# Two index lists in one tile of 96 bytes, and the buffers behind it on multiples of 128 bytes

## The reference

```python
for t in range(S):
    state = alpha[:, :, t, :, None] * state + np.einsum('bhd,bhe->bhde', k[:, :, t], v[:, :, t])
    y[:, :, t] = np.einsum('bhd,bhde->bhe', q[:, :, t], state)
...
for e in range(E):
    mask = expert_idx == e
    h = np.maximum(x[mask] @ w1[e], 0.0)          # 384 -> 1024
    out[mask] = gate_w[mask, None] * (h @ w2[e])  # 1024 -> 384
...
h = x @ w_in                                      # 384 -> 2048
g = np.maximum(0.01 * h, h)
return (g @ w_out).astype(np.float32)             # 2048 -> 384
```

## Time and profile before

| | us |
|---|---|
| median of 3 runs (lowest, highest) | 817.68 (817.54, 819.99) |
| span of the profiled execution, first to last instruction | 817.2 |
| TensorE matmul busy | 801.6 (98%) |
| VectorE, ScalarE, GpSimd busy | 452.1, 346.0, 209.0 |
| TensorE granted clock, share of full speed | 0.998 |

### The profile page before, as it was taken

How to read it: one execution, slowest core, us unless ns; L and a number is a source line. 1 busy time by engine, 2 the same in 40 slices (tenths; PEclk the granted TensorE clock), 3 DMA queues, 4 the chain that set the end, 5 groups by cost and what they waited for, 6 DMA issues and landing times.

```text
span 817.2 us, 17577 instructions
## 1 busy us (share of the span) xinstructions
PE 801.6 (98%) x5259; PEld 719.7 (88%) x5260; DVE 452.1 (55%) x705; ACT 346.0 (42%) x643; POOL 209.0 (26%) x278
## 2 busy tenths in 40 slices
PE   7899999999999999999999999999999999999998
PEld 7788887889989989999889988889998888998987
DVE  7899987686577476566565334433433533433332
ACT  3455554565446256444443333332333333334223
POOL 6567632223343343341241021003003001001000
PEclk9999999999999999999999999999999999999999
DMA  9988762777887887897741110201201001000001
GB/s 222 256 250 248 219 225 85 265 231 278 301 290 250 283 271 225 291 312 228 201 45 21 20 39 1 40 1 39 39 0 39 0 0 39 1 1 20 20 1 39
DMA packets 64130, 108.98 MB, mean 133 GB/s; under 512 B 24199, under 2 KB 45747, under 8 KB 64080
## 3 DMA queue, kind: packets, MB, share of 16 engines
q1 hardware_dynamic: 54896, 93.47, 37.7%
q0 software_dynamic: 5888, 14.85, 5.8%
q10 hardware_dynamic: 3296, 0.06, 0.2%
HBM read 78.89 MB, written 30.85 MB: 134 GB/s over the span
## 4 chain that ended last, share of the span: by engine, by line
PE 90%; DVE 3%; DMA 3%; issue 2%; POOL 1%; ACT 0%; DVEq 0%; ACTq 0%; SPq 0%; POOLq 0%
PE bank L1772 25%; PE bank L1721 24%; PE bank L1694 15%; PE bank L1674 14%; DMA qkas<-qka 2%; PE bank L1516 2%; PE bank L1556 2%; PE bank L1533 2%; PE bank L1564 1%; PE bank L1650 1%; PE bank L1522 1%; PE bank L1576 1%; POOL kt L675 1%; DVE decay L1073 0%; DMA xg<-x_rows,slot_src 0%
## 5 line engine op out<-in xcount | busy, mean ns | idle before, releaser
L1721 PE MATMUL bank<-yT,wts 128*128 128x512 f32 x864 | 217.5, 395 | 0.3 <-DVE yT L1306 0.3
L1772 PE MATMUL bank<-wts,gs 128*128 128x384 f32 x1152 | 215.5, 335 | 0.4 <-ACT os L1023 0.2
L1772 PEld LDWEIGHTS bank<-wts,gs 128*128 128x128 f32 x1152 | 202.0, 188 | 10.9 <-issue 2.0
L1721 PEld LDWEIGHTS bank<-yT,wts 128*128 128x128 f32 x864 | 160.6, 188 | 31.4 <-DVE yT L1306 1.0
L1302 DVE TENSOR_TENSOR g<-bank,small 128x512 f32<-128x512 f32 x96 | 66.4, 691 | 173.9 <-ACT small L929 163.8
L929 ACT ACTIVATE small<-bank 128x512 f32<-128x512 f32 x96 | 57.6, 600 | 184.8 <-PE bank L1721 170.3
L1674 PE MATMUL bank<-wts,gxT 128*128 (+1 forms) x549 | 133.5, 396 | 0.2
L1674 PEld LDWEIGHTS bank<-wts,gxT 128*128 128x128 f32 x549 | 100.8, 188 | 20.8 <-issue 0.8
L1483 DVE TENSOR_TENSOR gs<-g,gs 128x512 fp32r<-128x512 f32 x96 | 66.5, 693 | 66.8 <-ACT gs L1034 61.5
L1034 ACT ACTIVATE gs<-g 128x512 fp32r<-128x512 f32 x96 | 60.8, 633 | 78.0 <-DVE g L1302 71.3
L774 POOL DMA_INDIRECT out<-os,tokens x20 | 19.7, 986 | 288.1 <-ACT os L1023 283.5
(11 more groups left out here) (179 smaller groups left out, 768.4 us busy)
## 6 DMA issues: line engine op xcount, KB each, us to landing
raw<-weights SPq DMA_DIRECT2D x60, 512.0 KB
hidden_rows<-hs SPq DMA_DIRECT2D x29, 512.0 KB
hds<-hidden_rows SPq DMA_DIRECT2D x29, 512.0 KB
qkas<-qka SPq DMA_DIRECT2D x20, 675.5 KB, 5.1
vs<-v SPq DMA_DIRECT2D x24, 192.0 KB, 3.8
x_rows<-xs SPq DMA_DIRECT2D x24, 192.0 KB, 3.7
yl<-y_rows SPq DMA_DIRECT2D x20, 192.0 KB
qkas<-qka SPq DMA_DIRECT2D x4, 227.5 KB, 6.4
```

The costliest lines, as they stand in the source:

```text
L1721: m = pe.matmul(gps[f % 2][:, :], wts[:, 0, w_part, n:n + P], yT[:, 1 - u, y_part, k], start=(k == 0 and (w_part, y_part) == (0, 0)), stop ...
L1772: m = pe.matmul(ops[tt], gs[:, f % 4, g_part, tt * P:(tt + 1) * P], wts[:, 1, w_part, f * D:(f + 1) * D], start=(f == 0 and (g_part, w_par ...
```

## The change

The two lists become two pieces of one tile of 24 words (96 bytes). `isrc` is its words 0 and 1, `idst` its words 8 and 9, 32 bytes further on, so both stay at the very bytes at which they were. The tile is 32 bytes longer than the two slots were, and so every tile behind it moves up by 32 bytes: `yl`, `yf`, `yT` (now at byte 185,856), `hds`, `hr`, `os`, `hT_odd` and `tokens` now begin at multiples of 128 bytes, `row_gates` at 64 after one. An assertion holds `yT` there. No instruction is added, removed or moved on any engine; only addresses in instructions and DMA descriptors differ.

```diff
             ys = sb("ys", [P, 2, YW])
-            isrc = sb("isrc", [P, 2], I32)
-            idst = sb("idst", [P, 2], I32)
+            index = sb("index", [P, 24], I32)
+            isrc, idst = index[:, 0:2], index[:, 8:10]
             yl = sb("yl", [P, 2, GT // SQ, PIECE])
             yf = sb("yf", [P, 2, GT])
             yT_at = (nc.sbuf_base + 31) // 32 * 32
...
-            assert 3 * F <= 2 * KD * GT
+            assert 3 * F <= 2 * KD * GT and yT_at % P == 0
             os_at = (nc.sbuf_base + 31) // 32 * 32
             os_ = sb("os", [P, 2, TG, D])
```

## The result

The changed kernel takes 819.40 us (median of 22 runs, 817.39 to 823.57), the kernel before 817.78 us (22 runs): a ratio of 1.0023, 95% interval 1.0013 to 1.0032. It is slower, by 1.1 to 2.6 us. The forecast was 5.1 us faster, and the measured time lies above its whole range of 811.8 to 817.9 us. The profiled execution took 819.47 us with a span of 817.5, so what lies around a span is 2.0 us. The 0.5 us that the prediction took came from holding one execution's span against another's median.

A forecast was written before the change was run, and what follows sets the result against it. The prediction took TensorE's own pace, busy 98%, as the bound. Its terms, -5.34 us for `yT` and +0.28 for `hT_odd`, sum to -5.1: span 817.2 to 812.1, plus 0.5 gives 812.6 us, range 811.8 to 817.9.

The forecast's parts named there:

- What bounds the kernel: Whole kernel: TensorE's matmuls are busy 98% of the span, so only a change in TensorE's own pace matters.
- The pace and the 6.7 ns a matmul on top: Second network: `inner` takes 233.3 ns a matmul, `hidden` 226.7, both nines of 512 columns; 0.06 us more per nine.
- The step that failed: In `inner`: `yT` streaming from 96 bytes after a multiple of 128 touches one further 64-byte block, costing 6.7 ns a matmul.
- The term of -5.34 us: `yT` on a multiple of 128: `inner` falls from 2.10 to 2.04 us, 89 nines at 0.060 us less.
- `hT_odd`: Loaded operand of `contract`: once aligned, its 14 windows take the duration of `hT_even`, 0.02 us more each, 0.28 us more.
- The bound "0 and 0.3": Bounds in us on the cost of moving `hT_odd` in `contract`, from the rows with `hT_odd` and `hT_even`.
- ScalarE, VectorE, the list tile: Other engines and index lists: 96 bytes make no difference to ScalarE and VectorE, no row over 5 ns; lists cost 0.
- the start-up on both sides: Rival: adjacent aligned `inner` and `outward` runs both get a start-up, nearly cancelling the gain; about 817.5 us, chance 0.11.
- The slower rival: Loads and streams meet in SBUF: `inner` keeps 2.10 us, each `outward` gains 0.03 us; about 820.8 us, chance 0.07.
- The rule of 16-byte cachelines: Operand reads: starts at any multiple of 16 bytes cross equally many lines, so the `yT` term is 0; 817.9 us.
- 817.68 + 0.28: Rival of no change in `inner`: the 20 ns are not due to the address; about 817.9 us, chance 0.16.
- all 96 nines without the second term: Lower end, 811.8 us, of the clean case's range: every `inner` gains and `hT_odd` costs nothing; clean case's chance 0.52.

The follow-up runs named there:

- the map: Separate program, no reference computed: chains of 20 fp32r matmuls, 512 or 384 columns, at streamed-minus-loaded distances in 32-byte steps; excess 0.0 to 7.6 ns a matmul.
- the slower kernel above: Changed kernel with an index tile of 128 bytes instead of 96, everything behind it 64 bytes behind its earlier place; median 820.57 us, ratio 1.0036 against the kernel before.

## Why the prediction was wrong

- **What bounds the kernel**: right. TensorE alone decides; in every variant timed over ten runs or more the sum of its chains accounts for the time within its interval.
- **The pace and the 6.7 ns a matmul on top**: right as a reading of the earlier trace rows, but the two nines are not alike in what runs ahead of them. The nine of `hidden` follows nine matmuls of its own kind, `inner` an `outward`. With `inner` at distance 0 as well it still took 2.081 us and not 2.04: of the 0.060 us, 0.041 stayed.
- **The step that failed** is "I take the start of the streamed operand for the cause". The support was that 6.7 ns are 16 columns, one block of 64 bytes. The map shows an excess of 6.5 to 7.6 ns at six distances, two of them (128 and 192) with no such split block. What counts in steady chains is the distance between what is loaded and what is streamed, modulo 256, and in rounds also the chain ahead. `inner` went from 96 to 128, two places that both cost (7.5 and 6.7 ns in the map, 6.4 and 5.8 with a shifted load), and in rounds from 2,100 to 2,103 ns. The term of -5.34 us was +0.27, and `outward`, priced at nothing, added 0.28.
- **`hT_odd`**: the sign was right and the size was not, 0.98 us instead of 0.28. The step assumed that at a multiple of 128 it would be like `hT_even`; but `hT_even` lies 128 after a multiple of 256, like the weights, and `hT_odd` came to lie on one. The bound "0 and 0.3" was taken from the only two placements in the trace, and the new one was a third. The earlier trace rows held the clue: the displaced tile was faster.
- **ScalarE, VectorE, the list tile**: right. The rows of both engines in the second network moved by 2 ns at most; the only group of over four instructions that moved by more than 5 ns is ScalarE's fp32r piece of `wts` (1,052 to 1,046 ns), a tile that did not move. `inner` and `contract` stand as before with the list tile alone. TensorE's one listed wait for a transfer is 1.2 us in both traces.
- **The rivals**: the start-up on both sides is real, at 0.041 us left in the nine and 0.026 added to the twelve, but it did not come with this change. In the runs it comes to `outward` behind an `inner` at distance 0 and, in the slower kernel above, at 160 (2.109 us), not at 96 or 128. The slower rival had the right suspicion, loads and streams that depend on each other, with the wrong place: "equal placement makes them meet". Distance 0 is the best steady one for 512 columns, and the 0.03 us that this rival puts on each `outward` was 0.003: its direction came true by luck, its 820.8 us did not.
- **The rule of 16-byte cachelines** (the Trainium skill, "SBUF — State Buffer", section "Specifications (TRN2)") gave 817.9 us by the prediction's reading, 1.5 us under the measured time and nearer than the forecast. It is not the reason, and here the measurement decides: shifts by 32 bytes, all multiples of 16, change the pace by up to 7.6 ns a matmul.
- **Two small sums**: 817.68 + 0.28 is 818.0, not 817.9, and all 96 nines without the second term give 811.9, not 811.8. Neither matters.

What stays open is the mechanism inside: why the period is 256 bytes, why the rhythm changes with the width of the load, and why a start-up of 26 ns appears at distance 0 in 384 columns after some chains and not after others. No run here looked below the starts of matmuls.

## What to carry to other kernels

Where TensorE is busy all the time, read its pace from start to start per chain, and compare chains of the same shape: a few ns a matmul are a few us here. Place operands by pairs, not each by itself, and measure the placement in the rotation in which it runs, since a chain's start depends on the chain ahead; a small program with the same rounds predicted the whole kernel's round within 1 ns. Let such a program run several rounds of each placement and compare them, since some alternate. Two placements in a trace are two points of a curve, and a third needs a wider range than their difference.

## What the runs showed of the hardware

- In these runs fp32r matmuls with a fresh load of 128 columns run at their columns at 2.4 GHz plus 13.3 ns at best (226.7 ns for 512, 173.3 for 384).
- On top come 0 to 7.6 ns by the distance of streamed and loaded operand modulo 256 bytes, up to 3.4% of a matmul of 512 columns. The same within 0.1 ns at 256 bytes more, within about 1 ns with both operands shifted by 32 to 96 bytes.
- 384 columns have more clean distances (0 after a start-up, 32, 64, 160, 224) than 512 (0 only).
- A round of 9 matmuls of 512 and 12 of 384 columns lies between 4,147 and 4,227 ns by placement alone; 13 of 64 placements do not settle on one value in four rounds.
